# A fused attention and feed-forward kernel: early loads issued in pairs, and the first weight matrix in column halves

## The reference

```python
# 1. a decayed linear attention, B=2, H=8, S=768, head_dim=48; state starts at 0
for t in range(S):
    cur   = einsum('bhd,bhe->bhde', u * k_t, v_t)
    y_t   = einsum('bhd,bhde->bhe', r_t, state + cur)
    state = w_t[..., None] * state + einsum('bhd,bhe->bhde', k_t, v_t)
# 2. x: (2, 768, 384).  w1: 384 x 1536, w2: 1536 x 384
x = x + relu(layernorm(x) * g @ w1) @ w2
# 3. w_in: 384 x 1024, w_spatial: 768 x 768, w_out: 512 x 384
h = relu(x @ w_in); u, v = h[..., :512], h[..., 512:]
out = (u * (w_spatial @ normed(v) + b_spatial)) @ w_out
```

## Time and profile before

| | us |
|---|---|
| median of three timed runs | 433.31 |
| the profiled execution | 434.89 |
| its span, first to last instruction | 433.1 |
| TensorE busy in the span | 401.7 (93%) |
| VectorE busy | 223.0 (51%) |
| ScalarE busy | 147.5 (34%) |
| GpSimd busy | 126.9 (29%) |
| mean granted TensorE clock | 0.972 |

### The profile page before, as it was taken

One profiled execution on the slowest core, in us unless ns is written; L12 is line 12 of the kernel. 1 busy time (PEld: TensorE's weight loads), 2 busy tenths in 40 slices (PEclk: granted clock), 3 DMA queues, 4 the chain that ended last, 5 costly groups with the idle time before them and its releaser, 6 DMA issues.

```text
span 433.1 us, 12371 instructions
## 1 busy us (share of the span) xinstructions
PE 401.7 (93%) x5260; PEld 373.5 (86%) x5260; DVE 223.0 (51%) x492; ACT 147.5 (34%) x328; POOL 126.9 (29%) x149
## 2 busy tenths in 40 slices
PE   2477887999999999999999899999999999999997
PEld 2465776999999999999999799999988888989897
DVE  2488879856667666657543344133236934312120
ACT  3223454353442323232324322222227712211111
POOL 3376668736442423323220431001014500000000
PEclk9998866999999999999999899999999999999999
DMA  7914324503201020110000200000060100010102
GB/s 197 330 36 130 107 91 141 166 11 121 72 24 52 21 61 10 37 60 2 3 2 3 73 2 0 2 0 2 0 219 12 62 0 0 2 54 19 38 20 91
DMA packets 26555, 24.60 MB, mean 57 GB/s; under 512 B 1666, under 2 KB 23426, under 8 KB 26500
## 3 DMA queue, kind: packets, MB, share of 16 engines
q1 hardware_dynamic: 26500, 23.80, 17.8%
HBM read 21.44 MB, written 2.36 MB: 55 GB/s over the span
## 4 chain that ended last, share of the span: by engine, by line
PE 88%; DVE 4%; issue 3%; POOL 2%; DMA 1%; ACT 1%; SPq 0%; DVEq 0%; POOLq 0%; ACTq 0%
PE bank L1200 13%; PE bank L1202 11%; PE bank L1201 11%; PE low_bank L1119 9%; PE low_bank L1200 6%; PE low_bank L1202 6%; PE low_bank L1201 6%; PE high_bank L1200 4%; PE high_bank L1201 4%; PE high_bank L1202 4%; PE bank L1167 3%; PE bank L1163 2%; PE low_bank L1083 2%; PE bank L1194 2%; DVE near L863 1%
## 5 line engine op out<-in xcount | busy, mean ns | idle before, releaser
L556 POOL TENSOR_TENSOR kin<-kin,wtot 128x256 f32<-128x256 f32 x60 | 48.8, 820 | 67.9 <-PE low_bank L1119 66.0
L1119 PEld LDWEIGHTS low_bank<-rin,kin 64*64 64x64 f32 x2048 | 39.6, 149 | 28.8 <-issue 13.7
L1119 PE MATMUL low_bank<-rin,kin 64*64 64x32 f32 x2048 | 45.1, 233 | 20.6 <-DVE near L863 8.6
L821 DVE TENSOR_TENSOR rin<-rin,wtot 128x256 f32<-128x256 f32 x60 | 36.5, 612 | 14.5 <-PE low_bank L1119 13.6
L951 DVE SCALAR_TENSOR_TENSOR h10l<-bank,h10h 128x384 fp32r<-128x384 f32 x24 | 13.4, 558 | 43.6 <-ACT h10h L695 43.6
L863 DVE COPY_PREDICATED near<-msk,low_bank 128x256 f32<-128x256 int32 x64 | 32.7, 555 | 1.4 <-PE low_bank L1083 1.4
L554 POOL TENSOR_TENSOR kin<-kin,win 128x256 f32<-128x256 f32 x12 | 12.9, 1077 | 53.1 <-PE low_bank L1119 48.9
L573 POOL TENSOR_TENSOR vrstd<-vmv,half 128x1 f32<-128x1 f32 x12 | 7.7, 644 | 70.8 <-DVE vmv L1036 70.8
L1200 PE MATMUL bank<-xnT0h,ffw 128*128 128x384 f32 x66 | 24.5, 372 | 0.0
L695 ACT ACTIVATE h11h<-bank 128x384 fp32r<-128x384 f32 x16 | 7.9, 492 | 47.7 <-PE bank L1202 47.7
L1202 PE MATMUL bank<-xnT0h,ffw 128*128 128x384 f32 x66 | 22.5, 341 | 0.0
(11 more groups left out here) (242 smaller groups left out, 1134.0 us busy)
## 6 DMA issues: line engine op xcount, KB each, us to landing
kin<-in_kT SPq DMA_DIRECT2D x12, 256.0 KB, 3.4
rin<-in_rT SPq DMA_DIRECT2D x12, 256.0 KB, 4.8
win<-in_wT SPq DMA_DIRECT2D x12, 256.0 KB, 4.3
early_stage<-in_w SPq DMA_DIRECT2D x8, 384.0 KB, 5.1
vin<-in_v SPq DMA_DIRECT2D x12, 192.0 KB, 4.0
out<-ob SPq DMA_DIRECT2D x12, 192.0 KB, 1.9
stage<-in_w SPq DMA_DIRECT2D x4, 384.0 KB, 5.6
stage<-in_w_in SPq DMA_DIRECT2D x4, 384.0 KB, 3.6
```

The lines of the kernel that those rows point to most:

```text
L556: last = gp.tensor_tensor(k, k, wr[:, :, :, None].to_broadcast([P, NPR, m, c]), ALU.mult)
L821: last = ve.tensor_tensor(r, r, wl[:, :, :, None].to_broadcast([P, NPR, m, c]), ALU.mult)
L1119: mm = te.matmul(dst[s0:s0 + Q, NPR * e + a, :], kin[i % 4][lo:hi, a, s0:s0 + Q], r[:, :, 1, :], start=True, stop=True)
```

## The change

The six chunks of w1 are cut in another order: chunks 0 to 2 are the first column half (768 columns) of the three row blocks, chunks 3 to 5 the second half. Block 0 of the first product waits only for chunks 0 to 2, block 6 for all. All six w1 chunks are now loaded among the early loads. In these, almost every load waits until the load two places ahead of it has landed. The slots of the high and low parts of w1 move: both halves of chunk 0 fall in slot 0, and the later ones are spread out. The w2 chunks keep their splitting slots and are loaded two slots earlier.

```diff
-        for src, dst in ((w1, w1s), (w2, w2s), (w_in, wins), (w_sp, wsps), (w_out, wouts)):
+        for a in [k * F1 + h for h in range(0, F1, STAGE) for k in range(KC)]:
+            chunks.append((w1[:, a:a + STAGE], w1s[0][:, a:a + STAGE], w1s[1][:, a:a + STAGE]))
+        for src, dst in ((w2, w2s), (w_in, wins), (w_sp, wsps), (w_out, wouts)):
...
+        def chunk_loaded(eng, n):
+            eng.wait_ge(chunk_in_sbuf[slot_of[n]], 16 * loads_of_slot(n))
...
+        LO_SLOTS = [(0, 0), (2, 3), (4, 5), (7, 9), (12, 14), (17, 19)]
+
+        def lo_slots(n):
+            m = n - N_W1
+            return LO_SLOTS[n] if m < 0 else (SLOT_F1 - 2 + 2 * m, SLOT_F1 - 1 + 2 * m)
+
         def hi_slots(n):
-            m = n - W1C // STAGE
-            return [1 + 3 * n, 2 + 3 * n] if m < 0 else [SLOT_F1 - 4 + 2 * m, SLOT_F1 - 3 + 2 * m]
-
-        def lo_slots(n):
-            return [k + 2 for k in hi_slots(n)]
+            return [max(k - (1 if n < KC else 2), 0) for k in lo_slots(n)]
 
         def load_slot(n):
-            m = n - W1C // STAGE
-            return 3 * n - 3 if m < 0 else SLOT_F1 - 6 + 2 * m
+            return SLOT_F1 - 8 + 2 * (n - N_W1)
...
+            load_chunk(0)
             for i in range(1, 4):
+                w_loaded(sp, i - 1)
                 load_w(i)
+                chunk_loaded(sp, 2 * i - 2)
                 load_k(i)
+                w_loaded(sp, i)
                 load_r(i)
+                k_loaded(sp, i)
                 load_v(i - 1)
-                if i < 3:
-                    load_chunk(i - 1)
+                r_loaded(sp, i)
+                load_chunk(2 * i - 1)
+                v_loaded(sp, i - 1)
+                if 2 * i < N_W1:
+                    load_chunk(2 * i)
...
-                for n in range(2, N_FF):
+                for n in range(N_W1, N_FF):
...
                 if n == 0:
-                    split_waits(te, W1C // STAGE - 1)
+                    split_waits(te, KC - 1)
+                if n == NF // 2:
+                    split_waits(te, N_W1 - 1)
```

More of the change, by code:

```diff
@@ L177, in rwkv_moe_kernel @@
         chunks = []
-        for src, dst in ((w1, w1s), (w2, w2s), (w_in, wins), (w_sp, wsps), (w_out, wouts)):
+        for a in [k * F1 + h for h in range(0, F1, STAGE) for k in range(KC)]:
+            chunks.append((w1[:, a:a + STAGE], w1s[0][:, a:a + STAGE], w1s[1][:, a:a + STAGE]))
+        for src, dst in ((w2, w2s), (w_in, wins), (w_sp, wsps), (w_out, wouts)):
             for a in range(0, src.shape[1], STAGE):
                 chunks.append((src[:, a:a + STAGE], dst[0][:, a:a + STAGE], dst[1][:, a:a + STAGE]))
+        N_W1 = W1C // STAGE
         N_FF = (W1C + W2C) // STAGE
@@ L381, in f1_of @@
             return k - SLOT_F1 if k >= SLOT_F1 else None
+        LO_SLOTS = [(0, 0), (2, 3), (4, 5), (7, 9), (12, 14), (17, 19)]
+        def lo_slots(n):
+            m = n - N_W1
+            return LO_SLOTS[n] if m < 0 else (SLOT_F1 - 2 + 2 * m, SLOT_F1 - 1 + 2 * m)
         def hi_slots(n):
-            m = n - W1C // STAGE
-            return [1 + 3 * n, 2 + 3 * n] if m < 0 else [SLOT_F1 - 4 + 2 * m, SLOT_F1 - 3 + 2 * m]
-        def lo_slots(n):
-            return [k + 2 for k in hi_slots(n)]
+            return [max(k - (1 if n < KC else 2), 0) for k in lo_slots(n)]
         def load_slot(n):
-            m = n - W1C // STAGE
-            return 3 * n - 3 if m < 0 else SLOT_F1 - 6 + 2 * m
+            return SLOT_F1 - 8 + 2 * (n - N_W1)
         def weight_parts(k, slots_of):
             for n in range(N_FF):
-                if k in slots_of(n):
-                    yield n, slots_of(n).index(k)
+                for part, slot in enumerate(slots_of(n)):
+                    if slot == k:
+                        yield n, part
         def ff_steps():
@@ L635, in weight_hi @@
             def weight_hi(n, part=None):
-                act.wait_ge(chunk_in_sbuf[slot_of[n]], 16 * loads_of_slot(n))
+                chunk_loaded(act, n)
                 cs = slice(0, STAGE) if part is None else slice(part * STAGE // 2, (part + 1) * STAGE // 2)
```

## The result

The changed kernel takes 435.73 us (median of six runs, 435.08 to 436.60) against 433.22 us before (431.77 to 433.43): ratio 1.0069, 95% interval 1.0045 to 1.0092 (the ratio on record, here and below, is not the quotient of the two medians, which is 1.0058). By the medians it is 2.5 us slower; the forecast was 435.2 us, 1.9 slower. Six more runs, in another set, gave 435.04 against 432.66, ratio 1.0070 (1.0047 to 1.0093). The profiled execution takes 435.73 us, its span is 433.9.

The account below looks back on a forecast made before the run. TensorE was taken to bound the kernel, busy from 76 us on, so only earlier shifts count. Terms +1.85 - 0.3 + 0.3 = +1.9 us gave 436.8 for the profiled execution, 435.2 for the median; range 431.8 to 438.4.

Parts of the forecast that it names:

- The chain of waits: Early loads on SP: w of tile 3 lands at 29.55, delaying VectorE's decay product of tiles 2 and 3 by 1.85 us.
- the 2 to 4 that were named: Sign of being right: VectorE idle 2 to 4 us ahead of a 128x512 decay product at 29 to 30 us.
- The r step behind it: VectorE's level-2 r step, after the decay product, no longer runs beside a GpSimd step: -0.3 us.
- The fetch stall: TensorE's instruction wait near 19.6 us, 2.82 us long, taken as gone with fewer loads in flight.
- GpSimd's low parts: Six low parts in slots 0 to 5 instead of two: slot 5 about 1.6 us earlier, not 2.8; spent in waiting.
- The burst in round 2: Loads issued together once SP leaves its waits near 35.3 us, beside the second instruction gap ahead of 38.88: +0.3 us.
- The slower rival: VectorE waits longer for w of tile 3, TensorE perhaps at its lower clock after the gap: about 438 us; chance 0.20.
- Column halves: First product's block 0 waits for three w1 chunks instead of six, block 6 for the rest: no gain.
- The later low parts: Low parts moved among slots 10 to 17 cost only beside VectorE's normalisation: zero, within 0.4 us each way.
- the earlier w2 loads: w2 chunks loaded two slots earlier: zero, under a TensorE always busy from slot 20.
- Carried to the end one for one: TensorE is busy from 76 us on, so any shift before then reaches the end by the same amount.
- The sum: +1.9 us on the profiled 434.89 gives 436.8; less 1.58, that execution's excess over the median, gives 435.2.

Follow-up runs that it names:

- waits alone: The kernel before with its own early loads, each now waiting for the one two ahead; 432.72 us against 433.03, ratio 0.9996.
- w3 behind k3: The changed kernel with the load of w of tile 3 issued after k of tile 3; 439.90 us, ratio 1.0167 to the kernel before.
- w3 behind w2: The changed kernel with the load of w of tile 3 issued right behind that of tile 2; 432.48 us, ratio 0.9991 to the kernel before.
- old slots: The changed kernel with w of tile 3 loaded right behind tile 2's and w1 split in the slots of before; 431.22 us, ratio 0.9972 to the kernel before.
- decay product later: The changed kernel with the decay product of tiles 2 and 3 two slots later in VectorE's list; 433.30 us, ratio 0.9995 to the kernel before.
- waits alone with w3 behind w2: The kernel before with waits between its early loads and w of tile 3 loaded right behind tile 2's; 432.93 us against 432.66, ratio 0.9996.

## Why the prediction was right, point by point

**The chain of waits: right, and the step that carried it.** Landings forecast at 8.95, 12.45, 15.25, 18.95, 22.45 and 25.25 are at about 8.8, 11.9, 14.4, 18.6, 21.7 and 24.7. So the row for k was a little high (3.1 us for 3.4), the one for a chunk low (chunk 2 took 4.2 for 3.6). w3 itself was issued 0.8 us earlier than worked out and took 5.2 us and not 3.7, with chunks 3 and 4 in flight ahead of it; together 30.3 for 29.55. In the second profile of the change, behind the same two chunks, it took 3.7 us and its product ran at 29.51, so the chunks alone do not explain the 5.2. The wait of 4.49 us lies a little outside the 2 to 4 that were named, the second one (3.57) inside. The product shifted by 2.6 us (forecast 1.85), level 3 by 2.1.

**The r step behind it: right.** It took 0.42 us in place of 0.89, as GpSimd was through.

**The fetch stall: gone, as taken, but its size was that of an unusual run.** 2.82 us is the longest of five profiles of kernels without the waits; the others are 1.43, 1.71, 1.71 and 1.99. The packet came at 18.0, 18.2, 18.5 and 19.3 there, at 19.9 in the profile that the prediction read, and between 16.1 and 17.9 in all profiles with waits, with 0.34 us of issue at most at this place. Beside the work, it starts 0.9 to 1.8 us ahead of level 0 of tile 1 in the profiles with waits, and from 0.2 ahead to 1.3 behind in the others; where there is a gap, TensorE goes on 2.3 to 2.7 us after the packet's start in either kind. The Trainium skill (DMA: Bandwidth & Descriptors, Queues, rings and completion order) has each DMA engine take turns between queues packet by packet; by that the gap should not depend on the number of loads in flight, and here it does. What delays the fetch (the sharing of the DMA engines, or a request that is made later) is not shown. Nor do the waits end such gaps elsewhere: 2.12 us ahead of 38.04 (waits alone), 1.50 ahead of 44.03 (w3 behind k3), 0.82 ahead of 30.88 (w3 behind w2). The two later profiles of the kernel before, with the shorter stalls, have level 3 at 27.9 and 28.0; against them the change costs 3 to 4 us there.

**GpSimd's low parts: hidden, as said, but mis-sized.** Level 1 of tile 1 came 3.0 us earlier than in the profile before, not 1.6: chunk 1 landed near 16.5 (17.45 in the sum), so the level-3 step of tile 0 ended at 19.2 and not 20.4. Between the two profiles of the change and the two later ones of before it is 0.8 to 1.3 us. The low parts delay level 3 once w3 is early (the run with the old slots), and not in the changed kernel, where w3 is later still.

**The burst in round 2: not as described.** SP came out of the chain at 35.7 (35.3 forecast), but no issue gap stands near 38 in the changed kernel's profile. Something else was slow there: the 32 products of a level took 1.08 us at 36.67 and again at 39.56, where they took 0.67 at 36.42 in the profile of the kernel before. In the second profile of the change they took 0.67 at 35.80. The slower rival has TensorE slow after a long gap; the runs do not bear that out: with w3 behind k3 the gap is the longest (7.66 us), and the products behind it took 0.67 at 39.28, with w3 behind w2 no gap between 17 and 40 is over 1.5 us, and they took 1.08 at 33.80 and 36.68. The clock column of the profile reads 1.00 in all these places and so does not explain the 1.08. From level 3 to the first product it is 47.7 and 47.6 us in the two profiles of the change and 47.3 to 47.4 in the three of before, so the net is near the +0.3 that the sum had, by another way than it gave.

**Column halves: zero, as said,** shown by their own run. The later low parts and the earlier w2 loads, zero in the sum too, are not separated by any run.

**"Carried to the end one for one": failed between the two profiles, and open for the medians.** The first product moved from 77.12 to 79.55, by 2.4 us, the end of the span only from 433.1 to 433.9. The stretches around 245 us of before and of after have the rest:

```profile
240.00:244.00 4.00, 2.11 (x14) 1.83 (x12) 1.97 (x6) 2.10 (x5) 2.00 (x1) 1.00 0.36 98
244.00:248.00 4.00, 3.92 (x17) 3.95 (x18) 1.14 (x3) 1.58 (x3) 0.00 (x0) 0.65 0.35 98
248.00:252.00 4.00, 4.00 (x24) 3.97 (x23) 0.89 (x3) 1.34 (x4) 1.83 (x1) 0.92 0.00 0
```

```profile
244.00:248.00 4.00, 2.03 (x15) 1.79 (x14) 1.60 (x5) 1.36 (x4) 1.99 (x1) 1.00 0.43 118
248.00:252.00 4.00, 4.00 (x26) 3.96 (x25) 1.40 (x4) 1.70 (x3) 1.84 (x1) 1.00 0.15 60
```

In both, TensorE waits 2.0 us for the last transposed tile. Before, the granted clock fell behind that gap (0.65 in the seventh column, which is TensorE's clock); after, it did not. From the first product to the end of the span it is 355.9 to 356.0 us in the profiles with the fall (three of the kernel before, waits alone, old slots) and 354.3 to 354.4 in the eight others: 1.55 us. The fall comes with waits and without, but all five profiles with it are among the seven with the old splitting slots of w1, and none among the six with the new ones. Whether it is an accident of the run or an effect of the slots, so few profiles cannot say. The mean clock of the timed runs points the same way, without settling it: it is 0.972 or less in a third of the 75 runs of the kernel before in the three sets (all three of its profiles with the fall have 0.972) and in none of the 12 of the changed one, but two profiles without the fall have 0.972 too (decay product later, and waits alone with w3 behind w2). The fall hides part of the loss when profiles are compared: at the first product the two profiles of the change (79.55, 78.60) stand 3.2 to 4.4 us behind the two later ones of before (75.15, 75.38), at the end of the span (433.9, 433.0 against 431.1, 431.3) 1.7 to 2.8 us. The medians are 2.4 and 2.5 apart, less than at the first product. So some of what the change costs ahead of 76 us may be hidden in them as well.

**The sum.** 435.2 forecast, 435.73 and 435.04 measured. It was the right mechanism in the right place, and the size is close partly by luck. The sum gives 436.8 for the profiled execution and then takes off 1.58, because the profile of before was that much over its median. But that profile was long ahead of the first product (77.12, against 75.15 and 75.38), 1.1 to 1.4 us of it in the stall of 2.82, which the wait for w3 covers; an execution of the changed kernel has no such excess, and its profile (435.73) is the median of its runs. What brought the 436.8 down is the fall of the clock, which the profile of before has and that of after has not: 434.89 + 2.43 (the shift of the first product, for 1.9 in the sum) - 1.55 = 435.77. So an unfounded 1.58 stood where an unforeseen 1.55 was.

## What to carry to other kernels

When a load is made to wait for another, write down the chain of landings to each load and put beside it the first instruction that needs it; with operations that cover several tiles, that is the load of the last tile they cover. Here six steps of some 3 us put one load 4.5 us behind the moment at which its user was ready, and moving that one load five places up the list gave the whole loss back. A stall read from one profile is one draw: take a second profile before a term of the sum rests on its length, and look for the clock's falls behind each gap before two spans are subtracted. And do not read the time from one early landmark: level 3 stood at 26.3 and at 30.2 in two kernels here whose times are 0.6 us apart.

## What the runs showed of the hardware that was not expected

An instruction fetch of 16 KB comes later in a crowd of loads on another queue: its packet started at 18.0 to 19.9 us with all loads issued at once, and at 16.1 to 17.9 with two or three in flight, before the same operation of the program. And behind one gap of 2.0 us of TensorE, late in the kernel and there in all thirteen profiles, the granted clock falls to 0.50 (the lower of its two levels, 1.2 of 2.4 GHz) in five of them, at a price of 1.55 us, three fifths of the difference that this change makes.
